# Routing in halves, reads ahead of the loop, a new order in the first expert, and one identity product behind each first output

## What is computed

```python
def _moe2_ref(x, w_skip, w_gate, w1, w2) -> np.ndarray:
    skip_score = x @ w_skip
    do_compute = skip_score > 0
    out = x.copy()
    xc = x[do_compute]
    logits = xc @ w_gate
    e_idx = np.argmax(logits, axis=1)
    ...
    gate_w = probs[np.arange(len(xc)), e_idx]
    for e in range(E):
        mask = e_idx == e
        h = np.maximum(xc[mask] @ w1[e], 0.0)
        y[mask] = gate_w[mask, None] * (h @ w2[e])
    out[do_compute] = xc + y
    return out.astype(np.float32)
```

## Time and profile before

| what | us |
|---|---|
| median of 3 runs | 319.0 |
| lowest and highest | 317.29, 320.63 |
| the profiled execution | 317.01 |
| its span, first to last instruction | 315.3 |
| span busy on PE, DVE, ACT, POOL | 94%, 60%, 26%, 19% |
| mean granted clock of PE | 0.96 |

### The profile page before, as it was taken

One profiled execution on the slowest core, in us unless ns is written; L12 is line 12 of the kernel. 1 busy time (PEld: TensorE's weight loads), 2 busy tenths in 40 slices (PEclk: granted clock), 3 DMA queues, 4 the chain that ended last, 5 costly groups with the idle time before them and its releaser, 6 DMA issues.

```text
span 315.3 us, 8707 instructions
## 1 busy us (share of the span) xinstructions
PE 297.4 (94%) x3212; PEld 247.8 (79%) x3213; DVE 188.3 (60%) x436; ACT 83.5 (26%) x174; POOL 58.4 (19%) x62
## 2 busy tenths in 40 slices
PE   7699999999999999699998968999999999999995
PEld 7587887888887877563555746899999999999994
DVE  4799988989989894762232573626235262523523
ACT  1023223133231333132212372522231222223120
POOL 2685555453663310000000000000000000000000
PEclk9899999999999999999999575999999999999999
DMA  6999988869979889979999069700202020020202
GB/s 162 263 243 269 256 263 223 248 230 253 267 225 259 303 296 428 390 280 425 407 351 359 12 217 391 295 2 26 75 0 100 0 100 0 12 88 0 100 0 100
DMA packets 31312, 62.39 MB, mean 198 GB/s; under 512 B 4912, under 2 KB 22960, under 8 KB 30256
## 3 DMA queue, kind: packets, MB, share of 16 engines
q1 hardware_dynamic: 27824, 56.70, 53.8%
q10 hardware_dynamic: 3456, 5.25, 6.1%
HBM read 52.49 MB, written 9.44 MB: 196 GB/s over the span
## 4 chain that ended last, share of the span: by engine, by line
PE 85%; DVE 6%; issue 3%; DMA 2%; SPq 1%; ACT 1%; DVEq 0%; ACTq 0%
PE ps L1362 11%; PE ps L1364 10%; PE ps L1363 10%; PE ps L1099 8%; PE ps L1043 8%; PE ps L1122 4%; PE ps L1063 4%; PE ps L1345 4%; PE ps L1232 3%; PE ps L1251 3%; PE ps L1130 3%; PE ps L1322 3%; PE ps L1111 3%; PE ps L1075 3%; PE ps L1299 2%
## 5 line engine op out<-in xcount | busy, mean ns | idle before, releaser
L824 DVE SCALAR_TENSOR_TENSOR h_lo<-ps,h_hi 128x512 fp32r<-128x512 f32 x48 | 32.6, 691 | 63.1 <-ACT h_hi L991 63.1
L1362 PE MATMUL ps<-w_hi,h_hi 128*128 128x384 f32 x192 | 64.6, 337 | 0.2 <-issue 0.2
L1364 PE MATMUL ps<-w_hi,h_lo 128*128 128x384 f32 x192 | 64.5, 336 | 0.0
L1363 PE MATMUL ps<-w_lo,h_hi 128*128 128x384 f32 x192 | 64.5, 336 | 0.0
L991 ACT ACTIVATE h_hi<-ps 128x512 fp32r<-128x512 f32 x48 | 28.1, 598 | 79.0 <-PE ps L1345 74.2
L540 POOL TENSOR_TENSOR kt<-raw,dec_k 128x512 f32<-128x512 f32 x24 | 34.0, 1416 | 49.9 <-DMA raw<-rT 44.3
L1362 PEld LDWEIGHTS ps<-w_hi,h_hi 128*128 128x128 f32 x192 | 36.0, 188 | 1.9 <-issue 0.6
L1363 PEld LDWEIGHTS ps<-w_lo,h_hi 128*128 128x128 f32 x192 | 36.1, 188 | 1.6
L1364 PEld LDWEIGHTS ps<-w_hi,h_lo 128*128 128x128 f32 x192 | 36.1, 188 | 0.0
L646 DVE TENSOR_TENSOR at<-ps,mask 128x1024 f32<-128x1024 f32 x24 | 29.2, 1215 | 0.9 <-PE ps L1043 0.8
L1043 PE MATMUL ps<-rt,kt 48*128 48x128 f32 x384 | 28.6, 289 | 1.0 <-DVE at L646 0.7
(11 more groups left out here) (180 smaller groups left out, 368.4 us busy)
## 6 DMA issues: line engine op xcount, KB each, us to landing
w_first<-w1a SPq DMA_DIRECT2D x8, 768.0 KB, 5.1
w_first<-w2a SPq DMA_DIRECT2D x8, 768.0 KB, 6.9
a_slot<-w1a SPq DMA_DIRECT2D x4, 1536.0 KB, 13.7
x_slot<-w2a SPq DMA_DIRECT2D x3, 1536.0 KB, 10.7
out<-x SPq DMA_DIRECT2D x1, 4608.0 KB, 17.4
out<-x SPq DMA_DIRECT2D x24, 192.0 KB, 1.9
kn<-k_nat SPq DMA_DIRECT2D x20, 192.0 KB, 3.9
vn<-v_nat SPq DMA_DIRECT2D x20, 192.0 KB, 5.1
```

What stands on the lines that cost most here:

```text
L824: dve.scalar_tensor_tensor(out=h_lo[f % HB][:], in0=bank[4 + f % HB], scalar=0.0, in1=h_hi[f % HB][:].bitcast(F32), op0=ALU.max, op1=ALU.s ...
L1362: pe.matmul(bank[t][:, 0:DM], hh, w2_hi[:, f, :], start=(f == 0), stop=False)
L1363: pe.matmul(bank[t][:, 0:DM], hh, w2_lo[:, f, :], start=False, stop=False)
L1364: last = pe.matmul(bank[t][:, 0:DM], hl, w2_hi[:, f, :], start=False, stop=(f == FT - 1))
```

## The change

In words:

- `combine_by_slot(5)` goes into the middle of `second_layer(1)`. DVE does `low_of_c(5)` ahead of `take_so_t(1)`, and ACT does `high_of_c(5)` ahead of `take_so(1)`. Two `keep_warm` products stand behind `out_by_channel(1)`.
- The routing logits go to two banks of 12 tiles each, and DVE routes each half when it is there; the count is two products. From the eleventh logit on, one first output follows every third logit: outputs 0 to 4.
- Each output from 5 on is followed by one `keep_warm(1, 7)`.
- `exp_flag` gets a column, is read at the end of an expert instead of its start, and has a semaphore of its own. `past_expert` comes before `any_flag`.
- PE reads `first_expert` behind output 14 and does quarter 0 there, reads `past_expert` behind 16 and `next_group` behind 18. ACT and DVE also read, and split quarter 0 and the first quarter of the second weights, between their last copies.
- In the first expert PE runs `hidden` 0 and 1, quarters 1 and 2, `second(0)`, quarter 3 and `hidden(2)`; the first group's loop goes on from there.
- DVE takes 4 instead of 5 outputs (17, 19, 21, 22). The sum behind the gate goes to POOL, all but the reciprocal.

The diff, cut to its core:

```diff
+    U_FIRST, U_COUNT, U_EXP = 15, 9, 10
+    U_EARLY, RL_EARLY, RL_EVERY = 5, 10, 3
+    RT = TILES // 2
...
-            return u not in (5, 15, 17, 19, 21)
+            return u not in (17, 19, 21, 22)
...
+        def rl_bank(h):
+            return bank[5 - h][:, 0:RT * NR]
...
+        def expert_range(eng):
+            first = eng.value_load(first_expert[0:1, 0:1], min_val=0, max_val=E - 1)
+            eng.wait_ge(flags, 2)
+            past = eng.value_load(past_expert[0:1, 0:1], min_val=0, max_val=E)
+            return first, past
+
+        def routed_work(eng, expert, group, first, past):
...
-                with when_any(eng, exp_flag[0:1, bass.ds(e, 1)]):
+                with eng.If(eng.snap(has) > 0):
                     expert(e, eng.snap(ne), eng.snap(ng))
...
+                eng.wait_ge(exp_flagged, 1)
+                eng.reg_mov(has, eng.value_load(exp_flag[0:1, bass.ds(e + 1, 1)], min_val=0, max_val=1))
...
@@ vector engine @@
+            for h in range(2):
+                tiles = slice(h * RT, (h + 1) * RT)
+                rl = rl_bank(h).rearrange("p (u r) -> p u r", r=NR)
+                dve.wait_ge(rl_done, h + 1)
...
-            dve.wait_ge(count_done, 1)
+            dve.wait_ge(count_done, 2)
...
+            e_first, e_past = expert_range(dve)
+            take_x2(by_vector[0])
+            low_of_g(0)
+            for u in by_vector[1:-1]:
                 take_x2(u)
+            low_of_w2(0, e_first)
+            take_x2(by_vector[-1])
+            dve.wait_ge(gate_sum, 4)
+            dve.reciprocal(rs1[:], rs1[:]).then_inc(gate_sum, 1)
...
@@ scalar engine @@
+            for u in by_scalar_first:
+                take_x2(u)
+                if u == U_EXP:
+                    act.wait_ge(route_shift, 2)
                     act.activation(ra[:], ra[:], ACT.Exp).then_inc(route_exp, 1)
+            act.wait_ge(first_known, 1)
+            e_first, e_past = expert_range(act)
+            take_x2(by_scalar_last[0])
+            take_x2(by_scalar_last[1])
+            high_of_g(0)
+            take_x2(by_scalar_last[2])
+            act.wait_ge(w2q_in, 16 * FQ)
+            high_of_w2(0, e_first)
...
@@ tensor engine @@
-            second_layer(1)
-            combine_by_slot(5)
+            second_layer(1, lambda: combine_by_slot(5))
             out_by_channel(1)
+            pe.wait_ge(c4_ready, GROUPS)
+            keep_warm(2, 6)
...
                 pe.matmul(bank[u % 4][:, 0:DM], c4[:, u * P:(u + 1) * P], so4[:, 0:DM], start=True, stop=True).then_inc(x2_done, 1)
+                if u >= U_EARLY:
+                    keep_warm(1, 7)
+
+            for u in range(TILES):
+                last = pe.matmul(rl_bank(u // RT)[:, u % RT * NR:(u % RT + 1) * NR], c4[:, u * P:(u + 1) * P], so4[:, DM:DM + NR],
+                                 start=True, stop=True)
+                if u % RT == RT - 1:
+                    last.then_inc(rl_done, 1)
+                if u == RL_EARLY:
+                    pe.wait_ge(so4_ready, 2)
+                if u >= RL_EARLY and (u - RL_EARLY) % RL_EVERY == 0:
+                    first_output((u - RL_EARLY) // RL_EVERY)
...
+            for u in range(U_EARLY, U_COUNT):
+                if u == U_COUNT - 2:
+                    count(0)
                 first_output(u)
+            count(1)
+            for u in range(U_COUNT, U_FIRST):
+                first_output(u)
...
+            pe.wait_ge(first_known, 1)
+            e_first = pe.value_load(first_expert[0:1, 0:1], min_val=0, max_val=E - 1)
+            slot_hidden(0, e_first)
+            first_output(U_FIRST)
+            first_output(U_FIRST + 1)
+            pe.wait_ge(flags, 1)
+            e_past = pe.value_load(past_expert[0:1, 0:1], min_val=0, max_val=E)
+            first_output(U_FIRST + 2)
+            first_output(U_FIRST + 3)
             pe.wait_ge(left_ready, 1)
+            g_from, ng_from = pe.alloc_register("first_group"), pe.alloc_register("groups_ahead")
+            pe.reg_mov(g_from, group_left(e_first))
+            for u in range(U_FIRST + 4, TILES):
+                first_output(u)
+            pe.wait_ge(flags, 3)
...
+                pe.wait_ge(g4_ready, ne * GQ + 1)
+                start_group(start, ng)
                 pe.wait_ge(w1e_in[0], ne * 16 + 16)
+                slot_hidden(1, e)
                 pe.wait_ge(w1e_in[1], ne * 16 + 16)
+                slot_hidden(2, e)
                 pe.wait_ge(x2_act, n_scalar)
                 pe.wait_ge(x2_dve, TILES - n_scalar)
+                second(0, ng, ne)
+                pe.wait_ge(g4_ready, ne * GQ + 2)
+                slot_hidden(3, e)
+                pe.wait_ge(g4_ready, ne * GQ + 3)
+                hidden(2, start, ng)
```

More of the change, by code:

```diff
@@ L493, in _ @@
             sp.wait_ge(so_done, 2)
[L494 to L496 removed]
+            e_first = sp.value_load(first_expert[0:1, 0:1], min_val=0, max_val=E - 1)
+            load_expert(e_first)
+            sp.wait_ge(flags, 3)
+            e_past = sp.value_load(past_expert[0:1, 0:1], min_val=0, max_val=E)
+            ng = routed_work(sp, expert, group, e_first, e_past)
             with sp.If(sp.value_load(any_flag[0:1, 0:1], min_val=0, max_val=1) < 1):
@@ L801, in expert @@
             def expert(e, ne, ng):
[L802 to L811, removed]
-                low_of_g(0)
-                low_of_w2(0)
+                with dve.If(ne > 0):
+                    low_of_g(0, ne)
+                    low_of_w2(0, e, ne)
                 low_of_h(0, ng)
                 low_of_h(1, ng)
-                for k in range(1, GQ):
-                    low_of_g(k)
-                for k in range(1, WQ):
-                    low_of_w2(k)
+                low_of_g(1, ne)
+                low_of_g(2, ne)
+                low_of_w2(1, e, ne)
+                low_of_w2(2, e, ne)
+                low_of_g(3, ne)
+                low_of_w2(3, e, ne)
             def low_of_h(f, ng):
@@ L841, in group @@
                                              in1=row, op0=ALU.mult, op1=ALU.add).then_inc(y_added, 1)
-            routed_work(dve, expert, group)
+            routed_work(dve, expert, group, e_first, e_past)
         @block.scalar
@@ L959, in _ @@
+            act.wait_ge(first_known, 1)
[6 more added lines that the diff above has]
+            high_of_w2(0, e_first)
+            for u in by_scalar_last[3:]:
+                take_x2(u)
+            act.wait_ge(flags, 3)
             act.wait_ge(left_ready, 1)
-            act.wait_ge(w2q_in, 16 * FQ)
@@ L1001, in group @@
                 when_left(act, e, g + 1, start_next)
-            routed_work(act, expert, group)
+            routed_work(act, expert, group, e_first, e_past)
         @block.tensor
@@ L1247, in second_layer @@
                 for t in range(FT):
+                    if t == FH and midway is not None:
+                        midway()
                     for g in range(GE):
@@ L1285, in _ @@
             pe.wait_ge(c4_ready, GROUPS)
-            for u in range(TILES):
-                last = pe.matmul(bank[5][:, u * NR:(u + 1) * NR], c4[:, u * P:(u + 1) * P], so4[:, DM:DM + NR], start=True, stop=True)
-            last.then_inc(rl_done, 1)
-            pe.wait_ge(so4_ready, 2)
             taken = [0, 0]
@@ L1302, in _, with count @@
+            pe.sem_inc(g_done, 2)
+            def count(h):
+                pe.wait_ge(routed_ready, h + 1)
+                pe.matmul(bank[5][0:1, h * RT * E:(h + 1) * RT * E], ones_col[:],
+                          routed[:, h * RT:(h + 1) * RT].rearrange("p u e -> p (u e)"), start=True, stop=True).then_inc(count_done, 1)
+            for u in range(U_EARLY, U_COUNT):
+                if u == U_COUNT - 2:
+                    count(0)
                 first_output(u)
-            pe.sem_inc(g_done, 2)
@@ L1305, in _, with slot_hidden @@
-            pe.wait_ge(routed_ready, 1)
-            pe.matmul(bank[4][0:1, 0:TILES * E], ones_col[:], routed[:].rearrange("p u e -> p (u e)"), start=True, stop=True).then_inc(count_done, 1)
-            for u in range(6, TILES):
+            count(1)
+            for u in range(U_COUNT, U_FIRST):
                 first_output(u)
-            pe.wait_ge(w1q_in, 16 * KD)
-            pe.wait_ge(flags, 4)
-            pe.wait_ge(left_ready, 1)
+            def slot_hidden(q, e):
+                for k in range(KD):
+                    rhs = (w1q[:, k, bass.ds(e, 1), :].squeeze(1) if q == 0 else w1e[:, k, (q - 1) * FG:q * FG])
+                    last = pe.matmul(g_bank(q), so_t[:, k].rearrange("p r s -> p (r s)"), rhs,
+                                     start=(k == 0), stop=(k == KD - 1))
+                last.then_inc(g_done, 1)
@@ L1375, in group @@
                 when_left(pe, e, g + 1, lambda g_next: start_group(pe.snap(g_next * GN), ng + 1))
-                second(FT - 2)
-                second(FT - 1)
-            routed_work(pe, expert, group)
+                second(FT - 2, ng, ne - 1)
+                second(FT - 1, ng, ne - 1)
```

(1 more changed line is left out.)

178 lines of the change are left out of this document (93 added, 85 removed).

## The result

| | us |
|---|---|
| changed kernel, median of 20 runs | 315.52 (313.73 to 319.43) |
| kernel before, median of 20 runs | 317.63 (315.79 to 320.63) |
| ratio, with its 95% interval | 0.9944 (0.992 to 0.9969) |
| profiled execution of the changed kernel, and its span | 315.94, 314.2 |

The change wins 0.3 to 0.8%: the sign and the range of the forecast hold, its size does not. 5.0 us off the median of 319.0 were forecast; what came is 2.1 us off a median that twenty runs put at 317.63. (Medians here are over all timed runs, while ratios leave out runs more than 1.5% above the fastest of their kernel, which beside e5 to e8 takes away 11 of 35 runs of the kernel before but none of e5, e7 and e8, so that the ratios of these three come out 0.3 to 0.4% less favourable than their medians.)

A forecast was written before the change was run, and what follows sets the result against it. PE bounds the kernel (85% of the chain), at half clock for about 20 of the 30 us before the groups. -5.7 + 1.3 + 0.3 + 0.7 = -3.4 from 317.0 gives 313.6, set at 314.0 us; 8-in-10 range 310.0 to 318.5.

The forecast's parts named there:

- steps 1 to 7: From before the logits to the first expert: `second(0)` starts at 194.8 instead of 200.47, minus 5.7 us.
- Step 1: Before the logits: the combine moved into the second layer makes logits start 0.7 us later, at 173.6.
- Step 2: Logits and outputs 0 to 4: clock falls at 175.3, this part ends at 178.75.
- Steps 3 and 4: Routing of a half takes 1.9 us; outputs 5 to 14 and counts end at 185.1, clock rising at 183.0.
- Step 6: Quarter 0 and outputs 15 to 23: first two reads exposed 0.4 us each, third 0.5, quarter 1.3, end 191.0.
- Step 7: Into the expert: loop entry 0.7 us, two `hidden` 0.5, quarters 1 and 2 2.6, then `second(0)` at 194.8.
- step 8: Given back from `second(0)` on: quarter 3 plus 1.3 us, waits plus 0.3, SP's flag read at the end plus 0.7.
- The term for waits in the first group: Waits for `g4`, `hidden(2)` and its split behind the second weights: plus 0.3 us (0 to 1.0).
- The tail: Kernel end: SP must read `exp_flag` before `any_flag`, after its last store: plus 0.7 us.
- One fall instead of two: Clock before the groups: falls once between 174 and 177, back by 184.5, no half clock after 187.
- stays up: Rival at logits and outputs: identities and outputs between logits keep the clock at full, 311.1 us; chance 0.17.
- falls twice: Rival at 185 to 192: gaps from reads and waits bring a second fall, 3.6 more, 317.6 us; chance 0.19.

The follow-up runs named there:

- e5: Changed kernel with `exp_flag` allocated elsewhere, so `w2q`, `h_hi` and `h_lo` lie at the old addresses, no instruction different: median 315.80 us, ratio to before 0.9983.
- e8: Changed kernel with the repairs of e4 and e5 and SP's read of `any_flag` ahead of the loop: median 313.47 us, ratio to before 0.9909.
- e7: Changed kernel with the last combine behind the second layer again and the splits in their old order: median 317.89 us, ratio to before 1.0053.
- e4: Changed kernel with ACT and DVE taking the first group's `hidden(2)` ahead of the second weights' fourth part: median 314.90 us, ratio to before 0.9897.
- e6: Changed kernel with identity products also behind outputs 0 to 4 and the third, sixth and ninth logit: median 316.42 us.
- e1: Changed kernel without the identity product behind each first output: median 316.03 us, ratio to before 0.9981.
- e12: The kernel of e8 with no identity behind any output: median 312.86 us.
- e11: The kernel of e8 with identities only behind outputs 15 to 23: median 311.59 us, ratio to before 0.984.
- e3: Changed kernel with the first expert's old order, quarter 3 before the groups and `second(0)`, `hidden(2)` in the loop: median 314.93 us, ratio to before 0.9947.

## Why the prediction was right or wrong

- **The stretch (steps 1 to 7).** `second(0)` was put 31.0 us behind the layer's first product (194.8 - 163.8); it came at 29.49, in an execution with the shorter half clock (e5: 31.58). Step 1: the loss of 0.7 was 0.3. Step 2: the logits with outputs 0 to 4 take 4.05 instead of 5.15 us, since the clock fell 3.2 us after the first logit, not 1.7. Steps 3 and 4: the eight routing steps on 12 tiles took the 1.9 us forecast (176.51 to 178.38); outputs 5 to 14 with the counts take 7.7 (178.8 to 186.5) instead of 6.4 us, because the clock rose 6.0 us after dense work began, not 4.2. The price of a pair held, 0.75 at half clock and 0.40 (0.37 forecast) at full. Step 6: 4.9 us instead of 5.9: the reads, whose loads took 0.50, 0.32 and 0.31 us, were not exposed at all. PE's sequencer read beside queued products, with no issue gap ahead of quarter 0. Step 7: entry 0.5 instead of 0.7.
- **Given back (step 8), the step that failed.** The term for waits in the first group, 0.3 us with 1.0 as its upper end, measured 3.12 - 1.3 = 1.8. The sentence named the queue (second weights ahead of the split of `hidden(2)`) and not the read of `pair_flag` at the group loop's entry, which on DVE takes 0.92 us and with what goes with it some 1.5. e4 shows that 1.33 to 1.37 us of it was this wait. Some 0.14 us more are the addresses (first group 20.37 in e4, 20.23 in e8); 0.3 us stay open.
- **A term that was missing.** 0.73 us in the later groups, from 32 bytes (e5). The forecast put nothing for them and did not look at where tiles lie.
- **The tail.** +0.7 forecast, +0.64 measured; e8 won 0.58 of it back.
- **The clock.** One fall instead of two, as forecast; both clock rivals (stays up, falls twice) did not come about in the profile. In the changed kernel it fell at 178.0 with PE counted as busy throughout from 175 to 180 (and for 0.60 to 0.85 of each us from 171 to 175), and in the profiled execution of e6, with wider products in between, it stayed. By the Trainium skill's page "TensorE: Matmul & The Clock Gate", part 1 ("What's actually happening"), the clock follows how busy PE has been recently; taken by the profile's count of busy time, the fully busy us from 175 to 178 do not agree. But the falls of e5 and e7 at the first logit show that the work in front of the logits matters as well. And the importance given to the clock was too high: e1 and e12 have the second fall and are not measurably slower than their counterparts with identities.
- **The size.** -3.4 on the profiled execution became -1.1, or -2.7 without the front. The forecast of 314.0 was set against a median of three runs, 319.0, which made it a gain of 5; twenty runs put that median at 317.63, 0.6 above the profiled execution and not 2.0. The chance of 0.66 for a gain above 1% rested on it. The 2.9 us between the forecast gain of 5.0 and the 2.1 measured add up from the ledger's differences to the forecast, 1.5 (the wait of step 8), 0.7 (the later groups), 1.6 (the front) and -1.5 (the stretch), and 0.6 from the medians: the one before was taken as 2.0 us above its profiled execution and the new one as 0.4 above, and they are 0.6 above and 0.4 below.

## What to carry to other kernels

When work is moved forward in a list, follow it to its first consumer on every engine: a gain of 7.2 us at one mark was 2.7 us three marks on. Of the 4.5 us lost, 1.3 were a quarter moved on purpose, 1.4 a split that stood behind another split and a flag's read, 0.7 addresses and 0.6 a read at the end. A filler product costs twice as much where the clock is already low (0.43 against 0.22 us here), and behind an output at half clock it sets the pace (0.75 us a pair, where e11 needs 0.37 us for the output alone). Fillers at the gaps alone had the lowest median (e11); that they beat none at all (e12) is not shown. And compare tiles' addresses before and after a change that adds even one word to a small tile.

## What the hardware showed that was not expected

- 32 bytes of shift of `w2q`, `h_hi` and `h_lo` change the pace of the group products from 18.53 to 18.69 us (e5; of the other tiles only five small ones moved, which no product reads). Which of the three tiles does it was not tried.
- Reads into PE's registers cost PE nothing while products are queued, neither the three of 0.31 to 0.50 us between the outputs nor the first of `pair_flag`, which took 0.92 us at 196.7. The first read of `pair_flag` took as long on DVE (0.92 us at 200.15, against a median of 0.30), but there DVE's next split came behind it, and PE waited for the split.
- The half clock after the fall lasted 6.8 us both with identities (changed, e3, e8) and without (e1, e12), and in other executions 10.2 us both with all (e4, e5, e7) and with few (e11). It is not the same 10.2 us: with all identities the clock came back 18.5 to 19.9 us after the layer's first product in either case, and the longer half clock is one that began sooner (9.5 to 9.6 us after it instead of 11.7 to 12.6). In e11 it began at 12.5 and ended at 22.8.
- The clock can fall before the first thin product: in e7 at 173.8, 0.6 us before the first logit.
